# The second layer's activation in another form: h z / (z z + 1/4) over four tiles in flight

## What is computed

```python
x = attention(q, k, v, f_logit)            # 4 x 8 heads, 768 steps, head size 48
h = x @ w1_in;  x = (maximum(h, 0) ** 2) @ w1_out           # layer 1
h = x @ w2_in;  g = h * tanh(log(1 + exp(h)))               # layer 2
out = g @ w2_out                                            # float32
```

## Time and profile before

| | before |
|---|---|
| median of 3 runs | 976.34 us (975.35 to 976.48) |
| the profiled execution | 976.3 us, of which its span 974.3 us |
| mean granted TensorE clock | 0.982 |
| TensorE (PE) busy | 920.1 us (94%) |
| VectorE (DVE) busy | 630.6 us (65%) |
| ScalarE (ACT) busy | 534.8 us (55%) |
| GpSimd (POOL) busy | 190.2 us (20%) |

### The profile page before, as it was taken

The page is one execution under the profiler, slowest core; times in us unless marked ns, Lnnn a source line. Parts: engine busy times, 40 slices in busy tenths (PEclk is TensorE's granted clock), DMA queues, the critical chain, the costliest instruction groups (busy, mean ns, idle before and its releaser), DMA issues.

```text
span 974.3 us, 14347 instructions
## 1 busy us (share of the span) xinstructions
PE 920.1 (94%) x5248; PEld 768.8 (79%) x5248; DVE 630.6 (65%) x998; ACT 534.8 (55%) x951; POOL 190.2 (20%) x152
## 2 busy tenths in 40 slices
PE   3589999999999999999999999999999999999997
PEld 2468888888888888888787888888888888888886
DVE  5556533433433433332245999999999999999996
ACT  4466656556556555544566655555555554655544
POOL 3211111102111211110000232322323223232322
PEclk9589999999999999999999999999999999999999
DMA  6644514122321221301223201001001001000000
GB/s 183 182 125 124 176 28 122 45 78 78 89 78 50 73 69 54 94 9 42 86 94 114 66 1 33 33 1 33 33 1 33 33 1 33 34 1 1 34 1 32
DMA packets 42731, 58.38 MB, mean 60 GB/s; under 512 B 4130, under 2 KB 27682, under 8 KB 42658
## 3 DMA queue, kind: packets, MB, share of 16 engines
q1 hardware_dynamic: 42658, 57.43, 19.7%
HBM read 43.25 MB, written 14.16 MB: 59 GB/s over the span
## 4 chain that ended last, share of the span: by engine, by line
PE 51%; DVE 26%; ACT 11%; issue 9%; DMA 1%; POOL 0%; SPq 0%; DVEq 0%
PE ps L792 22%; PE ps L805 20%; DVE work L652 10%; DVE work L645 7%; DVE work L655 6%; ACT work L480 5%; ACT work L482 5%; PE ps L775 3%; PE ps L754 3%; PE ps L769 2%; DVE xs L623 1%; DVE g_lo L633 1%; PE ps L746 1%; PE ps L843 1%; DMA xs<-x_scratch 1%
## 5 line engine op out<-in xcount | busy, mean ns | idle before, releaser
L792 PE MATMUL ps<-xs,w_hi 128*128 128x512 f32 x1152 | 363.2, 396 | 12.6 <-DVE xs L623 11.7
L792 PEld LDWEIGHTS ps<-xs,w_hi 128*128 128x128 f32 x1152 | 212.0, 188 | 56.6 <-issue 13.1
L628 DVE TENSOR_TENSOR g_lo<-gb,g_hi 128x512 fp32r<-128x512 f32 x96 | 66.5, 692 | 255.1 <-ACT gb L451 255.1
L792 PE MATMUL ps<-xs,w_lo 128*128 128x512 f32 x576 | 227.3, 395 | 0.0
L394 POOL TENSOR_TENSOR work<-work 128x512 f32<-128x512 f32 x96 | 124.1, 1293 | 420.1 <-DVE work L645 420.1
L480 ACT ACTIVATE work<-work 128x512 f32<-128x512 f32 x96 | 60.8, 633 | 190.1 <-DVE work L655 190.1
L843 PE MATMUL ps<-w_hi,g_hi 128*128 128x384 f32 x384 | 136.8, 356 | 16.8 <-DVE g_lo L633 8.4
L446 ACT ACTIVATE rb<-ps 128x512 f32<-128x512 f32 x96 | 57.6, 600 | 143.6 <-PE ps L792 143.6
L843 PE MATMUL ps<-w_hi,g_lo 128*128 128x384 f32 x384 | 129.6, 337 | 0.0
L843 PE MATMUL ps<-w_lo,g_hi 128*128 128x384 f32 x384 | 129.6, 337 | 0.0
L792 PEld LDWEIGHTS ps<-xs,w_lo 128*128 128x128 f32 x576 | 108.4, 188 | 23.3
(11 more groups left out here) (57 smaller groups left out, 1154.5 us busy)
## 6 DMA issues: line engine op xcount, KB each, us to landing
work<-fkq SPq DMA_DIRECT2D x72, 224.0 KB, 4.0
xs<-x_scratch SPq DMA_DIRECT2D x12, 768.0 KB, 5.8
stage<-w_in SPq DMA_DIRECT2D x32, 192.0 KB, 2.4
stage<-w_out SPq DMA_DIRECT2D x32, 192.0 KB, 2.6
work<-v_tok SPq DMA_DIRECT2D x24, 192.0 KB, 3.1
x_scratch<-work SPq DMA_DIRECT2D x48, 96.0 KB, 2.1
x_scratch<-yo SPq DMA_DIRECT2D x6, 768.0 KB, 5.2
out<-work SPq DMA_DIRECT2D x24, 192.0 KB, 2.1
```

The costliest lines, as they stand in the source:

```text
L628: nc.vector.tensor_tensor(g_lo[:, t % 4, :], gb[:, t % 2, :], g_hi[:, t % 4, :].bitcast(F32), ALU.subtract).then_inc(s_["g1_ready"], 1)
L792: ins = nc.tensor.matmul(bank, w[:, f, k * P:(k + 1) * P], xs[:, half, part, k, :], start=k == 0 and i == 0, stop=k == KT - 1 and i == 2)
```

## The change

The same function is written with z = exp(-h) + 1/2: g = h z / (z z + 1/4). What is done per tile of layer 2 becomes this.

- ScalarE: exp(-h) (from PSUM), Square of z with a scale (new), Ln with the bias 1/4 (scaled by 2^-60), Exp with scale -1, and the copy for the high part.
- VectorE: one `tensor_scalar` (minimum and + 0.5), three `scalar_tensor_tensor` (`residual`, and two in `ratio`), one `tensor_tensor` that multiplies by h from PSUM (`g2`), and `g2_lo`.
- GpSimd: nothing. Its loop ends with the attention.

The tile z has four buffers instead of two. The order in a step becomes `residual(t - 2)`, `g2_lo(t - 3)`, `ratio(t - 2)`, `g2(t - 2)`, `shifted(t)` on VectorE, and on ScalarE it stays `g2_hi(t - 3)`, `reciprocal(t - 1)`, `exponential(t)`. `up2(t)` waits for `g2(t - 4)` (before: for L647 of tile t - 4, since that was the last reader of h). A tile of one column with the constant 1/4 is set at the start of the program, and two waits there count it.

```diff
-            for k in range(FIRST, 2 * NT + 1):
+            for k in range(FIRST, NT):
-                if 0 <= k - NT - 1 < NT:
-                    p_plus_mp(k - NT - 1)
+            def exponential(t):
+                act.wait_ge(s_["h2_done"], t + 1)
+                wait(act, s_["ratio2_ready"], t - 3)
+                nc.scalar.activation(zb[:, t % 4, :], ps_h2(t), ACT.Exp, scale=-1.0).then_inc(s_["e2_ready"], 1)
+            def reciprocal(t):
+                i = t % 2
+                act.wait_ge(s_["z2_ready"], t + 1)
+                wait(act, s_["r2_ready"], t - 1)
+                nc.scalar.activation(sb2[:, i, :], zb[:, t % 4, :], ACT.Square, scale=SCALE ** 0.5).then_inc(s_["s2_ready"], 1)
+                act.wait_ge(s_["s2_ready"], t + 1)
+                if t == 0:
+                    act.wait_ge(s_["set_up"], 4)
+                wait(act, s_["g2_raw"], t - 1)
+                nc.scalar.activation(rb2[:, i, :], sb2[:, i, :], ACT.Ln, bias=quarter[:, 0:1]).then_inc(s_["l2_ready"], 1)
+                act.wait_ge(s_["l2_ready"], t + 1)
+                nc.scalar.activation(rb2[:, i, :], rb2[:, i, :], ACT.Exp, scale=-1.0).then_inc(s_["p2_ready"], 1)
+            def shifted(t):
+                z = zb[:, t % 4, :]
+                dve.wait_ge(s_["e2_ready"], t + 1)
+                nc.vector.tensor_scalar(z, z, LARGEST, 0.5, ALU.min, ALU.add).then_inc(s_["z2_ready"], 1)
+            def residual(t):
+                i = t % 2
+                dve.wait_ge(s_["p2_ready"], t + 1)
+                nc.vector.scalar_tensor_tensor(out=sb2[:, i, :], in0=sb2[:, i, :], scalar=QUARTER, in1=rb2[:, i, :],
+                                               op0=ALU.add, op1=ALU.mult).then_inc(s_["t2_ready"], 1)
+            def ratio(t):
+                i = t % 2
+                r = rb2[:, i, :]
+                dve.wait_ge(s_["t2_ready"], t + 1)
+                nc.vector.scalar_tensor_tensor(out=r, in0=sb2[:, i, :], scalar=-2.0, in1=r,
+                                               op0=ALU.add, op1=ALU.mult).then_inc(s_["r2_ready"], 1)
+                dve.wait_ge(s_["r2_ready"], t + 1)
+                nc.vector.scalar_tensor_tensor(out=r, in0=r, scalar=SCALE, in1=zb[:, t % 4, :],
+                                               op0=ALU.mult, op1=ALU.mult).then_inc(s_["ratio2_ready"], 1)
+            def g2(t):
+                i = t % 2
+                dve.wait_ge(s_["ratio2_ready"], t + 1)
+                wait(dve, s_["g2_ready"], t - 1)
+                nc.vector.tensor_tensor(gb2[:, i, :], rb2[:, i, :], ps_h2(t), ALU.mult).then_inc(s_["g2_raw"], 1)
...
+                if 0 <= t - 2 < NT:
+                    residual(t - 2)
                 if 0 <= t - 3 < NT:
                     g2_lo(t - 3)
                 if 0 <= t - 2 < NT:
+                    ratio(t - 2)
                     g2(t - 2)
-                if 0 <= t - 1 < NT:
-                    products(t - 1)
                 if 0 <= t < NT:
-                    polynomial(t)
+                    shifted(t)
...
-                wait(pe, s_["hmp2_ready"], t - 3)
+                wait(pe, s_["g2_raw"], t - 3)
```

More of the change, by code:

```diff
@@ L33, in attention_ffn @@
     BOUND = 1.0e18
-    E20 = 485165195.40979028
+    SCALE = 2.0 ** -60
+    QUARTER = 2.0 ** -62
+    LARGEST = 2.0 ** 62
     PAR = [(0, D), (GAP, R)]
@@ L62, in attention_ffn @@
         pc = sb("pc", [P, 2, NP])
+        quarter = sb("quarter", [P, 1])
         mx = sb("mx", [P, 2])
@@ L110, in attention_ffn @@
         fsel, o = place(o, 2)
[L113 to L116, removed]
+        zb, o = place(0, 4, N)
+        sb2, o = place(o, 2, N)
+        rb2, o = place(o, 2, N)
+        gb2, o = place(o, 2, N)
         ob, o = place(o, B, DM)
@@ L160, in attention_ffn @@
             xs_hi xs_split h1_done r1_ready g1_hi g1_raw g1_ready g1_used o1_done o1_out x2_stored
-            h2_done u2_ready v2_ready m2_ready l2_ready p2_ready mp2_ready hmp2_ready pm2_ready g2_raw g2_hi
+            h2_done e2_ready z2_ready s2_ready l2_ready p2_ready t2_ready r2_ready ratio2_ready g2_raw g2_hi
             g2_ready g2_used o2_done o2_out o2_stored""".split()
@@ L473, in g2_hi @@
                 wait(act, s_["g2_used"], t - 3)
[L474 to L487, removed]
+                nc.scalar.activation(g_hi[:, t % 4, :], gb2[:, t % 2, :], ACT.Copy).then_inc(s_["g2_hi"], 1)
             def iteration(k):
@@ L563, in _ @@
             nc.vector.memset(ps[32:GAP, 5, :], 0.0).then_inc(s_["set_up"], 1)
-            dve.wait_ge(s_["set_up"], 3)
+            nc.vector.memset(quarter[:], QUARTER).then_inc(s_["set_up"], 1)
+            dve.wait_ge(s_["set_up"], 4)
             def scan(j):
@@ L631, in g2_lo @@
+            def g2(t):
[3 more added lines that the diff above has]
+                nc.vector.tensor_tensor(gb2[:, i, :], rb2[:, i, :], ps_h2(t), ALU.mult).then_inc(s_["g2_raw"], 1)
             def g2_lo(t):
                 dve.wait_ge(s_["g2_hi"], t + 1)
-                nc.vector.tensor_tensor(g_lo[:, t % 4, :], tb[:, t % 2, :], g_hi[:, t % 4, :].bitcast(F32),
+                nc.vector.tensor_tensor(g_lo[:, t % 4, :], gb2[:, t % 2, :], g_hi[:, t % 4, :].bitcast(F32),
@@ L634, in g2_lo @@
                                         ALU.subtract).then_inc(s_["g2_ready"], 1)
[L636 to L656, removed]
@@ L741, in scores @@
                     pe.wait_ge(s_["const_ready"], 2)
-                    pe.wait_ge(s_["set_up"], 3)
+                    pe.wait_ge(s_["set_up"], 4)
                 if was is not None:
```

## The result

| | before | after |
|---|---|---|
| median | 976.13 us (4 runs, 975.35 to 976.48) | 944.55 us (4 runs, 943.53 to 946.37) |
| ratio | | 0.968 (95% interval 0.9663 to 0.9696) |
| span of the profiled execution | 974.3 us | 941.8 us |

The forecast was 943.7 us with a span of 941.6. These rows stand on the page of the kernel after.

What follows compares the result with a forecast made beforehand. VectorE set layer 2's pace at 4.50 us a tile; TensorE was to take over at 4.19, with 90 tiles bringing `up2(95)` to 924.9, the last matmul to 938.4 and the span to 941.6: 943.7 us, range 939 to 953.

Steps and rivals of the forecast that it cites:

- VectorE's step: VectorE's instructions per tile of layer 2 after the change: 3.75 us from start to start, 3.85 on average with `x_lo`.
- The assumption on the unknown: Cost of `shifted` on VectorE in layer 2, unknown between 0.43 and 1.02 us; taken as 0.43, with GpSimd idle.
- ScalarE's step: ScalarE's work per tile of layer 2: 2.47 us before, 3.1 with the Square, 3.2 with hops, staying under VectorE.
- TensorE's pace: TensorE becomes layer 2's bound at 4.19 us a tile, read where nothing holds it, if its inputs are early.
- The two margins of 6 us: In layer 2, `g2(t)` ends 6 us before `up2(t + 4)` wants it, `g2_lo(t)` 6 us before `down2(t)` does.
- Chunk ends: First `down2` of a chunk waits 1.7 us for `out_rows`, five times, 8.4 us in all; taken as 0 after.
- The fill: Start of layer 2: `g2(0)` ends at 543.8, `up2(4)` waits 1.4 us, `up2(5)` starts at 548.05 instead of 547.30.
- The end: Last tile of layer 2: a 9.4 us chain from h to 936.5, last matmul at 938.4, then 3.24 to span end.
- A faster TensorE: Rival: TensorE's nine up products a tile run at layer 1's 0.2267 us, saving 0.04 us a tile; 940 us, 7%.
- The lasting wait at the chunk ends: Rival: ScalarE, with 0.6 us more work, is late at `out_rows`; 5 x 1.85 = 9.3 us, giving 953; 9%.
- the unchanged `shifted`: Rival: `shifted` still takes 1.02 us, VectorE stays the bound at 4.35 us a tile; about 962 us, 5%.
- The granted clock: Rival: waits in layer 2's tiles lower TensorE's clock for a fifth of its matmuls, adding 67 us; 1011 us, 3%.

Runs made afterwards that it cites:

- the order in pairs: The kernel after, with TensorE's order changed to two up products, then two down products; 942.39 us, ratio 0.9653.

## Why the prediction was right

**VectorE's step.** 3.75 us predicted, 3.60 measured in the step shown above. Five of the six terms agree within 0.02 us; `shifted` takes 0.33 from start to start, not 0.46, since `residual` of an older tile doesn't wait for it. One reading is slightly off: the five lines taken from rows 1 add up to 70%, not 71. The assumption on the unknown, 0.43 rather than 1.02 us, is the one that mattered, and the run without GpSimd's addition and the two runs with an added one show it for both kernels.

**ScalarE's step.** Here one term was mis-sized: the Ln was priced as before and takes 0.73, not 0.63. It is hidden, as the run with the bias 1.0 shows.

**TensorE's pace.** 4.187 us a tile was predicted from rows 8, and 4.187 is the median step after. No up or down product waited between 560 and 915 us. The two margins of 6 us can be read from the same trace: in the middle `g2(t)` ends 10.8 us and `g2_lo(t)` 12.9 us after `up2(t)` begins (predicted 10.6 and 12.8), which is 6.0 and 5.9 us before they are wanted. From tile 16 to tile 90 the margins never fall under 4.4 and 4.3. So the new wait of `up2` for `g2` was free, as argued.

**Chunk ends.** No wait after, as predicted. It came back with VectorE as the bound.

**The fill.** Predicted: `g2(0)` ends at 543.8, `up2(4)` waits 1.4 us, `up2(5)` starts at 548.05. Measured: 543.9, 1.32 and 548.27.

```profile
544.04 0.70 PE L802 MATMUL ps<-xs,w_hi 128*128 128x512 f32 x2 [1.32 <-DVE work L660]
...
548.27 0.63 PE L802 MATMUL ps<-xs,w_hi 128*128 128x512 f32 x2
```

**The end.** Predicted: the last `down2` starts at 936.5 after a wait of 1.2 us. In the chain (start us, us, what) it starts at 936.55.

```profile
927.35 0.61 ACT work L472
...
935.80 0.70 DVE g_lo L664
936.51 0.04 issue
936.55 2.37 PE ps L853 x12
```

That the two agree within 0.05 us is partly luck. The prediction's terms, 926.9 for the end of `up2(95)` and 9.4 for the chain, give 936.3 and not 936.5. The exponential started at 927.35, 0.45 later than that end, and the chain from there took 9.2. The wait of the last `down2` is 1.05 us (it starts at 936.55, and 0.174 behind the matmul before it would have been 935.50), where 1.2 was predicted.

**The rivals.** A faster TensorE fell: its up products kept 0.231 us. The lasting wait at the chunk ends and the unchanged `shifted` fell with the rows above. The granted clock was 1.00 over 575 to 915 us, and from 915 us to the end too, where before it was 0.50 from 965 to 967 us. The last digits owe something to chance, since the start of layer 2 alone moved between 532.0 and 535.4 us from run to run.

## What to carry to other kernels

Where an engine that sets the pace has one instruction much longer than its shortest case, look for what runs beside it: here 0.6 of 4.4 us were the blocking by an offloaded addition, as much as the addition would have cost on the engine itself. Moving an operation to an idle engine pays only until the next engine's pace is reached, so read that pace from a stretch where nothing holds it, and expect the gain to end there. Here 31.6 us came with the change of bound, and the fill and the order of TensorE's products gave 3.0 more.

## What the runs showed of the hardware

VectorE's `tensor_scalar` on 128x512 in SBUF takes 0.42 us with GpSimd idle, and 0.8 to 1.09 when GpSimd's addition of two SBUF tiles started before it, by how much of the addition was left. GpSimd's addition of two SBUF tiles takes 1.30 us beside VectorE's product with a PSUM tile and 1.74 us beside one that reads two SBUF tiles, and VectorE's own 0.69 doesn't change. An Ln with the bias from `quarter` and inputs scaled by 2^-60 took 0.726 us against 0.633. After a change from the 384-column to the 512-column form, matmuls followed at 0.231 us on average over nine, against 0.2267 in layer 1, with no regard to the load on the other engines; in the order in pairs they were back at 0.226 from the tenth on.
